# A fused attention, expert and gated kernel: the groups of small matmuls of two half-windows apart, and the loads placed otherwise in each slot

## The chip, the cores and the metric

The kernel runs on one core of a Trainium2 chip. The metric is the device time of one execution, in microseconds. Three runs of the kernel before took 1782.68, 1790.65 and 1793.02 us; the median is 1790.65 us. The profile is one more execution of its own.

## The reference

Three stages follow each other. Here they are, cut to what is computed:

```
q, k, v: (4, 8, 768, 48) float32, beta: (4, 8, 768)
# 1. delta-rule attention, for each of the 32 (batch, head) pairs, token after token
k_n = k / (norm(k) + 1e-6)
y[t]  = q[t] @ state
state = state + beta[t] * outer(k_n[t], v[t] - k_n[t] @ state)      # state is 48 x 48
# 2. x = y with heads side by side: (3072, 384); four experts, w1 (4,384,1024), w2 (4,1024,384)
p = domain_probs / (sum(domain_probs) + 1e-9)
x = sum over e of p[:, e] * (relu(x @ w1[e]) @ w2[e])
# 3. gated layer, w_gate and w_val (384,1536), w_out (1536,384)
out = (sigmoid(x @ w_gate) * (x @ w_val)) @ w_out
```

## The kernel before

**Windows and slots.** The attention stage doesn't go token by token. It takes chunks of 128 tokens (six of them) and half of the 32 heads at a time: 12 windows of 16 heads. Within a window the 128 steps of the recurrence become a triangular system for each head, and its inverse is built up from blocks of 32, then 64, then 128 rows. `slot(w, ...)` writes down one order of steps, and each engine (`@block.tensor`, `vector`, `scalar`, `gpsimd`) runs through the same list and takes from it the steps that it has work in. Engines meet only at semaphores, so the list fixes the order within each engine, and an engine that waits holds up everything behind it on that engine.

**What one slot holds.** Four kinds of work lie in slot w:

- `lev(step, w, p, hf)`: the triangular inverse of window w, for the half hf (8 heads). `first`, `y0` to `y3` and `z0` to `z3` are groups of matmuls on 32x32 blocks in float16 (lines 747 to 777), `m32y` and `m32z` (783 to 794) also, and `m64y`, `m64z` (802, 808) work on 64x64 blocks. A y group of one half is 32 matmuls; a z group is 4 wider ones and 32 small ones. After a y group VectorE masks the result (line 617), after a z group ScalarE copies it (line 531 is the common copy helper) and VectorE transposes it (line 602); the next group of that half needs both. `blocks` and `quads` are copies on GpSimd.
- `rec(step, w-1, ..., o)`: the recurrence of the window before, for the half o: `z`, `u0`, `au_a`, `au_b`, `u2`, `y`, `s` (float32 matmuls, lines 818 to 871).
- `pre(step, w+1, ...)`: the next window's norms, transposes (`turn`, line 879) and products (`product`, line 887); `product_q` is that of window w.
- `moe(step, m, ...)`, m = w-2: the first half of expert 0's hidden layer for the tokens that are done. `up` (line 934, nine matmuls 256 wide for one of four tiles f), ScalarE's Relu (line 595), VectorE's low part (`low`, line 711), `down` (line 943, three matmuls 384 wide for each f and each of two token tiles), and `weigh` (line 718), in which VectorE multiplies a finished tile by its expert weight into `part_out`. Where m is negative, four plain float16 matmuls stand in for each `up` and `down` (line 922).

`both(step)` runs a tile group for half 0 and then at once for half 1. So on TensorE the groups come in pairs: `y0` half 0, `y0` half 1, then the next piece of other work.

**Waits around the expert part.** `up(f)` uses one of two PSUM banks, f mod 2. For f below 2 it waits until `weigh(m-1, f)` has read that bank (`part_done`). In the list `weigh(m-1, 1)` stands after `both("z0")` and ahead of `au_a`, and `up(1)` after `au_a`. There is one `part_out` place: each `weigh` waits until the store of the one before has landed (`part_stored`).

**The DMA queue.** All transfers are issued by SyncE (SP) in one order, in a loop over w: `load_v`, the store of one weighed part, `load_k`, `load_b` (beta, spread over the partitions), at w = 2 the second half of expert 0's weights, the two stores of y, `load_x` (it waits for the y stores to land and reads them back for the expert part), `load_q`, and the store of the other weighed part. A `wait_ge` in that loop holds back all that follows it. `up(0)` waits for `load_x`.

**After the 12 slots** a tail finishes the last windows, and then the experts (lines 1050 to 1178) and the gated layer (lines 1308 to 1414) run. The change doesn't touch them.

Of the kernel before, what the change touches and what calls it, by code (L numbers as in the profile page):

```python
# [7 lines left out]
F32 = mybir.dt.float32  # L8
# [6 lines left out]
P = 128  # L15
# [52 lines left out]
def delta_rule_attention(nc, q, k, v, beta, consts, places, x_hi, x_lo, ident, id_in, early):  # L68
# [9 lines left out]
    with ctx:  # L78
        def sb(name, shape, dt=F32):
            return ctx.enter_context(nc.sbuf_tensor(name, shape, dt))  # L80
# [48 lines left out]
        w2h = [sb(f"w2half_{part}", [P, KH, KD * P], F32R) for part in "hl"]  # L129
        xs = [sb(f"xs_{part}", [P, KD, 2, P], F32R) for part in "hl"]  # L130
        hs = [sb(f"hs_{part}", [P, KH, 2 * P], F32R) for part in "hl"]
        part_out = sb("part_out", [P, KD * P])

        w_split = sem("w_split")
        p_in = sem("p_in")
# [67 lines left out]
        def slot(w, p, lev, rec, pre, moe):  # L203

            m, has_next = w - 2, w < NW - 1

            def r(step, o):
                if w > 0 and not (step == "s" and w == NW - 1):
                    rec(step, w - 1, 1 - p, o)

            def n(step, which=None):
                if has_next:
                    pre(step, w + 1, 1 - p, which)

            def both(step):
                for hf in range(2):
                    lev(step, w, p, hf)

            def down(window, t, *fs):
                for f in fs:  # L220
                    moe("down", window, t, f)

            def up(f):
                for part in range(2):
                    moe("up", m, f, part)

            pre("value", w, p, None)
            n("square")
            both("first")
            moe("weigh", m - 1, 0)  # L230
            r("u0", 0)
            down(m - 1, 1, 0, 1)
            r("u0", 1)
            both("y0")
            n("norm")
            down(m - 1, 1, 2, 3)
            up(0)
            n("unit", 0)
            n("unit", 1)
            both("z0")  # L240
            moe("weigh", m - 1, 1)
            r("au_a", 0)
            moe("low", m, 0)
            up(1)
            both("y1")
            r("au_b", 0)
            moe("low", m, 1)
            up(2)
            both("z1")
            r("au_a", 1)  # L250
            rec("z", w, p, 0)
            moe("low", m, 2)
            both("y2")
            n("turn", 0)
            r("au_b", 1)
            n("turn", 1)
            both("z2")
            r("u2", 0)
            rec("z", w, p, 1)
            both("y3")  # L260
            n("product", 0)
            r("u2", 1)
            both("z3")
            both("blocks")
            both("quads")
            r("y", 0)
            both("m32y")
            up(3)
            n("product", 1)
            both("m32z")  # L270
            moe("low", m, 3)
            r("y", 1)
            pre("product_q", w, p, 0)
            both("m64y")
            r("s", 0)
            down(m, 0, 0, 1)
            pre("product_q", w, p, 1)
            both("m64z")
            r("s", 1)
            down(m, 0, 2, 3)  # L280
            n("turn_q", 0)
            n("turn_q", 1)

        def run(lev, rec, pre, moe):
# [59 lines left out]
        with nc.Block() as block:  # L344

            @block.sync
            def _(sp):
# [4 lines left out]
                def load_k(w):  # L352
                    sp.dma_start(k_raw[w % 2][:, :, :], rows_of(k, w // 2, w % 2)).then_inc(k_in[w % 2], 16)

                def load_v(w):
                    sp.dma_start(v_raw[:, :, :], rows_of(v, w // 2, w % 2)).then_inc(v_in, 16)
# [35 lines left out]
                def store_part(m, o):  # L392
                    tok = first_token(m, o)
                    sp.wait_ge(part_done, 2 * m + o + 1)
                    sp.dma_start(early.part[tok:tok + P, :], part_out[:, :]).then_inc(part_stored[o], 16)

                load_k(0)
                sp.dma_start(ident[:, :], consts[2]).then_inc(id_in, 16)
# [7 lines left out]
                load_k(1)  # L406
                load_b(1)
                load_q(1)
                sp.dma_start(early.probs_raw[:, :, :], early.probs).then_inc(p_in, 16)
                early.load_first(sp)  # L410
                for w in range(NW):
                    if w + 1 < NW:
                        sp.wait_ge(vb_done, w + 1)
                        load_v(w + 1)
                    if 3 <= w:
                        store_part(w - 3, 1)
                    if w + 2 < NW:
                        sp.wait_ge(ku_done, 2 * (w + 1))
                        load_k(w + 2)
                        sp.wait_ge(kb_done, 2 * (w + 1))  # L420
                        load_b(w + 2)
                    if w == 2:
                        sp.wait_ge(w_split, 4)
                        early.load_second(sp)
                    if w:
                        store_y(w - 1, 0)
                        store_y(w - 1, 1)
                        load_x(w - 1)
                    if w + 2 < NW:
                        sp.wait_ge(tq_rdy, 2 * (w + 1))  # L430
                        load_q(w + 2)
                    if 2 <= w:
                        store_part(w - 2, 0)
                store_part(NW - 3, 1)
                store_part(NW - 2, 0)
                store_y(NW - 1, 0)
                store_y(NW - 1, 1)
                load_x(NW - 1)
                store_part(NW - 2, 1)
                for o in range(2):  # L440
                    store_part(NW - 1, o)
                for o in range(2):
                    sp.wait_ge(y_out[o], 64 * NW)
                    sp.wait_ge(part_stored[o], 16 * NW)
# [155 lines left out]
            def _(dve):  # L600
# [106 lines left out]
                def moe(step, m, f, part=1):  # L707
                    if step == "low" and m >= 0:
                        dve.wait_ge(hh_done, KH * m + f + 1)
                        past(dve, dn_rdy, 2 * m)  # L710
                        nc.vector.scalar_tensor_tensor(out=hs[1][:, f, :], in0=ebank[f % 2][:, 0:2 * P], scalar=0.0,
                                                       in1=hs[0][:, f, :].bitcast(F32), op0=ALU.max,
                                                       op1=ALU.subtract).then_inc(hl_done, 1)
                    if step == "weigh" and m >= 0:
                        tile = (2 * (m % 2) + f) * NCH + m // 2
                        dve.wait_ge(dn_rdy, 2 * m + f + 1)
                        past(dve, part_stored[1 - f], 16 * (m + f))
                        nc.vector.tensor_scalar(part_out[:, :], ebank[f][:, 0:KD * P],
                                                early.weights[:, tile, 0:1], None, ALU.mult).then_inc(part_done, 1)

                nc.vector.memset(XTf[:, :, :].bitcast(F32), 0.0).then_inc(x_zeroed, 1)
# [229 lines left out]
class Early:  # L951


    def __init__(self, nc, ctx, w1, w2, probs, halves_raw):
        E, D, F = w1.shape
        N = probs.shape[0]
        self.nc, self.kd, self.kh = nc, D // P, F // P // 2
        self.raw1 = halves_raw[:, 0:self.kd * F // 2].rearrange("p (t f) -> p t f", f=F // 2)
        self.raw2 = halves_raw[:, self.kd * F // 2:].rearrange("p (t d) -> p t d", d=D)
        self.w1, self.w2 = w1[0].rearrange("(t p) f -> p t f", p=P), w2[0].rearrange("(t p) d -> p t d", p=P)  # L960
        self.probs = probs.rearrange("(t p) e -> p t e", p=P)
        self.raw_in = ctx.enter_context(nc.semaphore("halves_in"))
        self.probs_raw = ctx.enter_context(nc.sbuf_tensor("pr", [P, N // P, E], F32))
        self.weights = ctx.enter_context(nc.sbuf_tensor("pn", [P, N // P, E], F32))
        self.sums = ctx.enter_context(nc.sbuf_tensor("psum_p", [P, N // P], F32))
        self.guarded = ctx.enter_context(nc.sbuf_tensor("prec", [P, N // P], F32))
        self.part = nc.dram_tensor("part", (N, D), F32, kind="Internal").ap()

    def load(self, sp, n):
# [7 lines left out]
    def load_second(self, sp):  # L977
        self.load(sp, 1)

    def normalize(self, dve, p_in, p_steps):  # L980
        nc, pr, pn = self.nc, self.probs_raw, self.weights
        dve.wait_ge(p_in, 16)
        nc.vector.reduce_sum(self.sums[:, :], pr[:, :, :], AX_X).then_inc(p_steps, 1)
        dve.wait_ge(p_steps, 1)
        nc.vector.tensor_scalar(self.guarded[:, :], self.sums[:, :], 1e-9, None, ALU.add).then_inc(p_steps, 1)
        dve.wait_ge(p_steps, 2)
        nc.vector.reciprocal(self.sums[:, :], self.guarded[:, :]).then_inc(p_steps, 1)
        dve.wait_ge(p_steps, 3)
        nc.vector.tensor_tensor(pn[:, :, :], pr[:, :, :], self.sums[:, :].unsqueeze(2).to_broadcast(pn.shape),
                                ALU.mult).then_inc(p_steps, 1)  # L990
        dve.wait_ge(p_steps, 4)

# [534 lines left out]
```

## Time and profile before

| | us |
|---|---|
| median of 3 runs | 1790.65 |
| lowest and highest | 1782.68, 1793.02 |
| the profiled execution, whole | 1771.93 |
| its span from first to last instruction | 1770.1 |
| TensorE (PE) busy | 1687.9 |
| PE weight load (PEld) busy | 1516.4 |
| VectorE (DVE) busy | 621.7 |
| ScalarE (ACT) busy | 443.8 |
| GpSimd (POOL) busy | 206.5 |

The profiled execution stands apart from the three timed ones and was faster than each. Busy time counts a matmul from its start to its modelled end, and matmuls overlap, so it is not a measure of progress. Starts are: the distance from the start of one group to the start of the next is the time that a group takes on PE. A lower granted clock makes the same work take longer, and the page shows it in tenths for 40 slices. "issue" as a releaser stands for time in which the engine waited for nothing that the profile shows.

### The profile page before, as it was taken

How to read it: one execution, taken by the hardware profiler on the slowest of the kernel's cores; microseconds unless marked ns; L12 is line 12 of the kernel's file. 1: busy time of each engine (PE TensorE's matmuls, PEld its weight loads, DVE VectorE, ACT ScalarE, POOL GpSimd, SP SyncE). 2: the span in 40 equal slices, each digit the busy share in tenths (PEclk: the TensorE clock that was granted, in tenths of full speed). 3: DMA queues.
4: the chain of work that ended last, by engine and by line, in shares of the span. 5: the costliest groups of instructions: out<-in, count | busy, mean ns of one | idle time of the engine just before them, and what ended most of it. 6: DMA issues, size and time to landing. Idle time of an engine off the chain costs nothing. (4 is left out here: it accounts for less than half of the span.)

```text
span 1770.1 us, 41908 instructions
## 1 busy us (share of the span) xinstructions
PE 1687.9 (95%) x18182; PEld 1516.4 (86%) x18182; DVE 621.7 (35%) x1169; ACT 443.8 (25%) x852; POOL 206.5 (12%) x309
## 2 busy tenths in 40 slices
PE   2899999999997799999999999999989999999999
PEld 2788899888987689999999999999978888888887
DVE  2565666565653223222222222222244222222222
ACT  2333333333331121221112111111133222222222
POOL 2522222222230030030002100000000000000000
PEclk9998999898998899999999999999999999999999
DMA  7143333333213734112122112112012000000000
GB/s 152 32 113 87 87 86 87 86 86 86 66 48 89 260 107 166 47 36 71 36 107 71 36 36 98 36 36 71 0 64 71 19 0 19 18 0 18 0 19 18
DMA packets 171757, 113.68 MB, mean 64 GB/s; under 512 B 82224, under 2 KB 151216, under 8 KB 171600
## 3 DMA queue, kind: packets, MB, share of 16 engines
q1 hardware_dynamic: 171600, 111.33, 22.1%
q8 instruction: 129, 2.11, 0.5%
q14 instruction: 28, 0.23, 0.0%
HBM read 92.44 MB, written 18.87 MB: 63 GB/s over the span
## 5 line engine op out<-in xcount | busy, mean ns | idle before, releaser
L1149 DVE SCALAR_TENSOR_TENSOR hl<-ebank,hh 128x512 fp32r<-128x512 f32 x168 | 116.3, 692 | 506.4 <-ACT hh L1114 506.4
L1114 ACT ACTIVATE hh<-ebank 128x512 fp32r<-128x512 f32 x168 | 100.6, 599 | 582.2 <-PE ebank L1178 582.2
L1176 PE MATMUL ebank<-w2l,hh 128*128 128x384 f32 x672 | 226.5, 337 | 2.6 <-DVE hl L1149 2.6
L1178 PE MATMUL ebank<-w2h,hh 128*128 128x384 f32 x672 | 226.6, 337 | 0.0
L1177 PE MATMUL ebank<-w2h,hl 128*128 128x384 f32 x672 | 225.9, 336 | 0.0
L1176 PE MATMUL ebank<-xl,w1h 128*128 128x512 f32 x504 | 197.2, 391 | 10.1 <-DMA xl<-x_lo 10.1
L1178 PE MATMUL ebank<-xh,w1h 128*128 128x512 f32 x504 | 199.7, 396 | 0.0
L1177 PE MATMUL ebank<-xh,w1l 128*128 128x512 f32 x504 | 199.5, 396 | 0.0
L1176 PEld LDWEIGHTS ebank<-w2l,hh 128*128 128x128 f32 x672 | 126.4, 188 | 9.8 <-DVE hl L1149 3.1
L1177 PEld LDWEIGHTS ebank<-w2h,hl 128*128 128x128 f32 x672 | 126.4, 188 | 6.0
L1178 PEld LDWEIGHTS ebank<-w2h,hh 128*128 128x128 f32 x672 | 126.3, 188 | 0.0
L1372 DVE TENSOR_TENSOR prod<-gbank,gate 128x512 f32<-128x512 f32 x72 | 49.7, 690 | 209.3 <-ACT gate L1319 209.3
L1176 PEld LDWEIGHTS ebank<-xl,w1h 128*128 128x128 f32 x504 | 95.4, 189 | 26.5 <-DMA xl<-x_lo 10.4
L1178 PEld LDWEIGHTS ebank<-xh,w1h 128*128 128x128 f32 x504 | 95.1, 189 | 20.4
L1177 PEld LDWEIGHTS ebank<-xh,w1l 128*128 128x128 f32 x504 | 95.2, 189 | 16.7
L1406 PE MATMUL gbank<-wol,mh 128*128 128x384 f32 x288 | 98.4, 342 | 0.7 <-DVE ml L1376 0.7
L1408 PE MATMUL gbank<-woh,mh 128*128 128x384 f32 x288 | 97.1, 337 | 0.0
L1407 PE MATMUL gbank<-woh,ml 128*128 128x384 f32 x288 | 96.8, 336 | 0.0
L1319 ACT ACTIVATE gate<-gbank 128x512 f32<-128x512 f32 x72 | 43.0, 598 | 208.6 <-PE gbank L1408 208.6
L1406 PE MATMUL gbank<-gxl,wgh 128*128 128x512 f32 x216 | 84.8, 393 | 4.4 <-DVE gxl L1366 4.4
L1408 PE MATMUL gbank<-gxh,wgh 128*128 128x512 f32 x216 | 86.2, 399 | 0.0
L1407 PE MATMUL gbank<-gxh,wgl 128*128 128x512 f32 x216 | 86.0, 398 | 0.0
(160 smaller groups left out, 2914.9 us busy)
## 6 DMA issues: line engine op xcount, KB each, us to landing
xh<-x_hi SPq DMA_DIRECT2D x24, 768.0 KB, 4.4
xl<-x_lo SPq DMA_DIRECT2D x24, 768.0 KB, 6.0
brep<-in_beta SPq DMA_DIRECT2D x24, 256.0 KB, 5.4
k_raw<-in_k SPq DMA_DIRECT2D x12, 384.0 KB, 4.5
v_raw<-in_v SPq DMA_DIRECT2D x12, 384.0 KB, 4.5
q<-in_q SPq DMA_DIRECT2D x12, 384.0 KB, 5.7
x_hi<-yhi SPq DMA_DIRECT2D x48, 96.0 KB, 2.1
x_lo<-ylo SPq DMA_DIRECT2D x48, 96.0 KB, 2.2
```

The source lines that it names most:

```text
L1114: nc.scalar.activation(hs[i][0][:, :], bank[i][:, :], ACT.Relu).then_inc(hh_done, 1)
L1149: nc.vector.scalar_tensor_tensor(out=hs[i][1][:, :], in0=bank[i][:, :], scalar=0.0, in1=hs[i][0][:, :].bitcast(F32), op0=ALU.max, op1=ALU. ...
L1176: mm(dst, stat[0], mov[1], start=first, stop=False)
L1177: mm(dst, stat[1], mov[0], start=False, stop=False)
L1178: return mm(dst, stat[0], mov[0], start=False, stop=last)
L1319: nc.scalar.activation(gate[:, :], bank[f % 2][:, :], ACT.Sigmoid).then_inc(gate_done, 1)
L1372: nc.vector.tensor_tensor(prod[:, :], bank[2 + f % 2][:, :], gate[:, :], ALU.mult)\
L1406: mm(dst, stat[0], mov[1], start=first, stop=False)
L1407: mm(dst, stat[1], mov[0], start=False, stop=False)
L1408: return mm(dst, stat[0], mov[0], start=False, stop=last)
```

## The change

The pairs of tile groups are taken apart: behind each half stands a piece of other work. `weigh`, `low`, `norm` and `product` keep their places between the same groups as far as that goes, and so `weigh(m-1, 1)` now stands behind `z0` of half 1 and directly ahead of `up(1)`. `part_out` has two places, one for each half, and the scratch of the weight normalization lies in it. SP's loop has a new order. The diff, without the lines that only rename the normalization's scratch:

```
-        part_out = sb("part_out", [P, KD * P])
+        part_out = sb("part_out", [P, 2, KD * P])
+        early.room(part_out[:, :, :].rearrange("p t d -> p (t d)"))
...
-            def both(step):
-                for hf in range(2):
-                    lev(step, w, p, hf)
+            def tiles(step, hf):
+                lev(step, w, p, hf)
...
             n("square")
-            both("first")
+            tiles("first", 0)
+            r("u0", 0)
+            tiles("first", 1)
             moe("weigh", m - 1, 0)
-            r("u0", 0)
             down(m - 1, 1, 0, 1)
             r("u0", 1)
-            both("y0")
+            tiles("y0", 0)
+            down(m - 1, 1, 2, 3)
+            tiles("y0", 1)
             n("norm")
-            down(m - 1, 1, 2, 3)
             up(0)
             n("unit", 0)
             n("unit", 1)
-            both("z0")
+            tiles("z0", 0)
+            r("au_a", 0)
+            tiles("z0", 1)
             moe("weigh", m - 1, 1)
-            r("au_a", 0)
             moe("low", m, 0)
             up(1)
-            both("y1")
+            tiles("y1", 0)
             r("au_b", 0)
+            tiles("y1", 1)
             moe("low", m, 1)
             up(2)
-            both("z1")
+            tiles("z1", 0)
             r("au_a", 1)
+            tiles("z1", 1)
             rec("z", w, p, 0)
             moe("low", m, 2)
-            both("y2")
+            tiles("y2", 0)
             n("turn", 0)
             r("au_b", 1)
+            tiles("y2", 1)
             n("turn", 1)
-            both("z2")
+            tiles("z2", 0)
             r("u2", 0)
+            tiles("z2", 1)
             rec("z", w, p, 1)
-            both("y3")
+            tiles("y3", 0)
             n("product", 0)
+            tiles("y3", 1)
             r("u2", 1)
-            both("z3")
-            both("blocks")
-            both("quads")
+            tiles("z3", 0)
             r("y", 0)
-            both("m32y")
+            tiles("z3", 1)
+            tiles("blocks", 0)
+            tiles("blocks", 1)
+            tiles("quads", 0)
+            tiles("quads", 1)
             up(3)
+            tiles("m32y", 0)
             n("product", 1)
-            both("m32z")
+            tiles("m32y", 1)
             moe("low", m, 3)
             r("y", 1)
+            tiles("m32z", 0)
             pre("product_q", w, p, 0)
-            both("m64y")
+            tiles("m32z", 1)
             r("s", 0)
             down(m, 0, 0, 1)
+            tiles("m64y", 0)
             pre("product_q", w, p, 1)
-            both("m64z")
+            tiles("m64y", 1)
             r("s", 1)
-            down(m, 0, 2, 3)
+            down(m, 0, 2)
+            tiles("m64z", 0)
+            down(m, 0, 3)
             n("turn_q", 0)
+            tiles("m64z", 1)
             n("turn_q", 1)
...
                 for w in range(NW):
-                    if w + 1 < NW:
-                        sp.wait_ge(vb_done, w + 1)
-                        load_v(w + 1)
+                    if w:
+                        store_y(w - 1, 0)
                     if 3 <= w:
+                        store_part(w - 3, 0)
                         store_part(w - 3, 1)
                     if w + 2 < NW:
                         sp.wait_ge(ku_done, 2 * (w + 1))
                         load_k(w + 2)
+                    if w + 1 < NW:
+                        sp.wait_ge(vb_done, w + 1)
+                        load_v(w + 1)
+                    if w:
+                        store_y(w - 1, 1)
+                    if w + 2 < NW:
                         sp.wait_ge(kb_done, 2 * (w + 1))
                         load_b(w + 2)
-                    if w == 2:
-                        sp.wait_ge(w_split, 4)
-                        early.load_second(sp)
                     if w:
-                        store_y(w - 1, 0)
-                        store_y(w - 1, 1)
                         load_x(w - 1)
                     if w + 2 < NW:
                         sp.wait_ge(tq_rdy, 2 * (w + 1))
                         load_q(w + 2)
-                    if 2 <= w:
-                        store_part(w - 2, 0)
-                store_part(NW - 3, 1)
-                store_part(NW - 2, 0)
+                    if w == 2:
+                        sp.wait_ge(w_split, 4)
+                        early.load_second(sp)
+                for o in range(2):
+                    store_part(NW - 3, o)
                 store_y(NW - 1, 0)
                 store_y(NW - 1, 1)
                 load_x(NW - 1)
-                store_part(NW - 2, 1)
-                for o in range(2):
-                    store_part(NW - 1, o)
+                for m in (NW - 2, NW - 1):
+                    for o in range(2):
+                        store_part(m, o)
...
                     if step == "weigh" and m >= 0:
...
-                        past(dve, part_stored[1 - f], 16 * (m + f))
-                        nc.vector.tensor_scalar(part_out[:, :], ebank[f][:, 0:KD * P],
+                        past(dve, part_stored[f], 16 * m)
+                        nc.vector.tensor_scalar(part_out[:, f, :], ebank[f][:, 0:KD * P],
```

## Rows read from the trace of the kernel before

**Rows 1.** The page: engine totals, and the queue that carries instructions (packets, MB).

```profile
PE 1687.9 (95%) x18182; PEld 1516.4 (86%) x18182; DVE 621.7 (35%) x1169; ACT 443.8 (25%) x852; POOL 206.5 (12%) x309
...
q8 instruction: 129, 2.11, 0.5%
```

**Rows 2.** Windows, one for each of slots 2 to 10: stretch, busy, PEclk, DMA, GB/s.

```profile
core 0: us, PE busy (x) PEld busy (x) DVE busy (x) ACT busy (x) POOL busy (x), PEclk, DMA share, GB/s
114.52:160.45 45.93, 43.72 (x1034) 39.71 (x1033) 26.11 (x58) 16.42 (x36) 11.43 (x21) 0.89 0.44 112
...
284.74:325.38 40.64, 39.94 (x1029) 36.62 (x1028) 26.45 (x60) 16.14 (x36) 11.45 (x21) 1.00 0.41 92
325.38:372.15 46.77, 44.53 (x1030) 40.66 (x1029) 26.66 (x60) 16.25 (x36) 11.45 (x21) 0.89 0.38 86
...
413.23:460.57 47.34, 45.63 (x1030) 41.61 (x1030) 26.86 (x60) 16.47 (x36) 11.45 (x21) 0.86 0.34 80
460.57:501.21 40.64, 39.97 (x1030) 36.66 (x1030) 26.45 (x60) 16.14 (x36) 11.45 (x21) 1.00 0.29 67
sum 386.69, PE 374.35 PEld 341.92 DVE 238.49 ACT 145.94 POOL 103.04; mean PE 41.59 PEld 37.99 DVE 26.50 ACT 16.22 POOL 11.45
```

**Rows 3.** Waits of PE and its weight loads, 50 to 560 us: total, times, longest.

```profile
PE bank L934 <- DVE part_out L718: 4.4, 9, 0.5
...
PEld bank L887 <- DVE QK L704: 4.3, 11, 0.6
```

**Rows 4.** Timeline of PE in slot 4, groups merged: start, length, engine, line.

```profile
209.60 0.29 PE L772 MATMUL bank<-XX,c 32*32 32x256 f16 x4
...
210.02 0.29 PE L772 MATMUL bank<-XX,c 32*32 32x256 f16 x4
...
210.46 1.09 PE L841 MATMUL bank<-U,A 128*128 128x48 f32 x8
212.04 0.39 PE L934 MATMUL bank<-xs_l,w1half_h 128*128 128x256 f32 x1 [0.49 <-DVE part_out L718]
...
213.30 0.67 PE L763 MATMUL bank<-XX,Ah 32*32 32x32 f16 x64
213.89 1.09 PE L844 MATMUL bank<-U,A 128*128 128x48 f32 x8
...
222.79 1.07 PE L852 MATMUL bank<-R,XTf 128*128 128x48 f32 x8
223.70 1.11 PE L818 MATMUL bank<-S,KQ 128*128 128x96 f32 x8
...
226.43 1.07 PE L852 MATMUL bank<-R,XTf 128*128 128x48 f32 x8
227.44 0.29 PE L772 MATMUL bank<-XX,c 32*32 32x256 f16 x4
```

**Rows 5.** Timeline of PE in slot 0: a y half standing alone.

```profile
43.34 0.40 PE L763 MATMUL bank<-XX,Ah 32*32 32x32 f16 x32 [0.36 <-DVE XX L610]
43.67 3.59 PE L922 MATMUL bank<-c 128*128 128x256 f16 x16
```

**Rows 6.** Timeline of VectorE in slot 4, ahead of `up(1)`.

```profile
210.70 0.79 DVE L602 STREAM_TRANSPOSE XX<-XX 128x256 f16<-128x256 f16 x2 [1.80 <-ACT XX L531]
211.41 0.58 DVE L718 TENSOR_SCALAR part_out<-bank,pn 128x384 f32<-128x384 f32 x1
```

**Rows 7.** Timeline of PE: the longest stalls of slots 2, 7 and 9.

```profile
134.35 0.26 PE L772 MATMUL bank<-XX,c 32*32 32x256 f16 x1 [2.03 <-issue]
...
341.31 0.18 PE L777 MATMUL bank<-Yc,XX 32*32 32x32 f16 x1 [1.57 <-issue]
...
431.69 0.98 PE L844 MATMUL bank<-U,A 128*128 128x48 f32 x7 [1.04 <-issue]
```

**Rows 8.** Windows, columns as in Rows 2, ahead of the stall in slot 7.

```profile
336.00:340.00 4.00, 3.74 (x154) 3.38 (x152) 1.79 (x5) 1.15 (x3) 0.00 (x0) 1.00 0.91 202
```

**Rows 9.** Timeline of SP: a load issue of slot 7, and the x loads around slot 5's start.

```profile
335.64 1.98 SPq L366 DMA_DIRECT2D brep<-in_beta  x2
...
243.38 0.91 SPq L389 DMA_DIRECT2D xs_h<-x_hi  x2
```

More of the change, by code:

```diff
@@ L394, in store_part @@
                     sp.wait_ge(part_done, 2 * m + o + 1)
-                    sp.dma_start(early.part[tok:tok + P, :], part_out[:, :]).then_inc(part_stored[o], 16)
+                    sp.dma_start(early.part[tok:tok + P, :], part_out[:, o, :]).then_inc(part_stored[o], 16)
                 load_k(0)
@@ L408, in _ @@
                 load_q(1)
-                sp.dma_start(early.probs_raw[:, :, :], early.probs).then_inc(p_in, 16)
+                sp.dma_start(early.probs_raw, early.probs).then_inc(p_in, 16)
                 early.load_first(sp)
                 for w in range(NW):
-                    if w + 1 < NW:
-                        sp.wait_ge(vb_done, w + 1)
-                        load_v(w + 1)
+                    if w:
+                        store_y(w - 1, 0)
                     if 3 <= w:
+                        store_part(w - 3, 0)
                         store_part(w - 3, 1)
@@ L962, in __init__ @@
         self.raw_in = ctx.enter_context(nc.semaphore("halves_in"))
-        self.probs_raw = ctx.enter_context(nc.sbuf_tensor("pr", [P, N // P, E], F32))
         self.weights = ctx.enter_context(nc.sbuf_tensor("pn", [P, N // P, E], F32))
-        self.sums = ctx.enter_context(nc.sbuf_tensor("psum_p", [P, N // P], F32))
-        self.guarded = ctx.enter_context(nc.sbuf_tensor("prec", [P, N // P], F32))
         self.part = nc.dram_tensor("part", (N, D), F32, kind="Internal").ap()
@@ L978, in load_second, with room @@
         self.load(sp, 1)
+    def room(self, scratch):
+        n, e = self.weights.shape[1:]
+        self.probs_raw = scratch[:, 0:n * e].rearrange("p (n e) -> p n e", e=e)
+        self.sums, self.guarded = scratch[:, n * e:n * e + n], scratch[:, n * e + n:n * e + 2 * n]
     def normalize(self, dve, p_in, p_steps):
@@ L982, in normalize @@
         dve.wait_ge(p_in, 16)
-        nc.vector.reduce_sum(self.sums[:, :], pr[:, :, :], AX_X).then_inc(p_steps, 1)
+        nc.vector.reduce_sum(self.sums, pr, AX_X).then_inc(p_steps, 1)
         dve.wait_ge(p_steps, 1)
-        nc.vector.tensor_scalar(self.guarded[:, :], self.sums[:, :], 1e-9, None, ALU.add).then_inc(p_steps, 1)
+        nc.vector.tensor_scalar(self.guarded, self.sums, 1e-9, None, ALU.add).then_inc(p_steps, 1)
         dve.wait_ge(p_steps, 2)
-        nc.vector.reciprocal(self.sums[:, :], self.guarded[:, :]).then_inc(p_steps, 1)
+        nc.vector.reciprocal(self.sums, self.guarded).then_inc(p_steps, 1)
         dve.wait_ge(p_steps, 3)
-        nc.vector.tensor_tensor(pn[:, :, :], pr[:, :, :], self.sums[:, :].unsqueeze(2).to_broadcast(pn.shape),
+        nc.vector.tensor_tensor(pn[:, :, :], pr, self.sums.unsqueeze(2).to_broadcast(pn.shape),
                                 ALU.mult).then_inc(p_steps, 1)
```

## The prediction

> **What bounds the kernel now.** I first read the page's totals and then cut the attention stage into its slots. PE is busy for 95% of the span [rows 1], but ends of matmuls are modelled, so I read starts. By slots [rows 2], the reader is to see that the bare slot lasts 40.64 us (slots 6 and 10, PEclk 1.00), that its 1029 matmuls follow each other nearly without a hole, and that DVE (26.5), ACT (16.1) and POOL (11.5) have slack. So a slot is the sum of what PE does, and whatever the change adds to PE is paid in full. The nine slots together take 386.69 us, and nine bare ones would take 365.76: 20.9 us are disturbance, and 18.1 of them lie in three slots, 45.93, 46.77 and 47.34 us long, with a mean clock of 0.89, 0.89 and 0.86. The timeline shows in each of those a stall put down to "issue", of 2.03, 1.57 and 1.04 us [rows 7], and the slots' low clock comes after it. The stall is of the kind that late instructions would give: the page has 129 transfers of instructions, 2.11 MB or 16 KB each [rows 1], and ahead of the stall in slot 7 the DMA engines were 0.91 busy [rows 8] with the load of k and beta issued some 3.7 us before [rows 9]. Last, the table of waits [rows 3] names two small regular ones, on `weigh` (9 times, 0.5 us at most) and on QK's mask (11 times, 0.6 at most).
>
> **The change, part by part.**
>
> *Thirteen pairs of tile groups taken apart.* The same matmuls run, but the array goes between small tiles and full width 13 more times per slot, in and out. Both edges have a price in the starts. A pair of y groups takes 213.89 - 213.30 = 0.59 us [rows 4]; one alone took 0.33 [rows 5], two are 0.66: +0.07. In a z pair the first half takes 0.42 (210.02 - 209.60) and the second, which goes over to wide work, 0.44 [rows 4]: +0.02. And the piece put between ends before tiles: the same eight `u2` matmuls take 0.91 us ahead of wide work and 1.01 ahead of tiles [rows 4]: +0.10. So a split y costs 0.17 and a split z or `first` 0.12. Four y, four z, `first`: 0.68 + 0.48 + 0.12 = 1.28 us. For `m32y`, `m32z`, `m64y`, `m64z` I have no single half; between 0.02 (z's own edge) and 0.17, and since they are bare groups as y is, 0.13 each, 0.5 together. Some pieces put between (`product`, `y` of the recurrence) are followed by another shape in both orders, so that about four of the 0.10 fall away: -0.4. I take 1.4 us per slot. Bounds: 0.4 if only y's and z's trailing edges counted (4 x 0.07 + 5 x 0.02), 13 x 0.17 = 2.2 if each cost the most. Twelve slots: 17 us (5 to 26).
>
> The Trainium skill (TensorEngine Tiling (Array Packing), Tiling Modes, Key Properties) says that changing the tiling mode drains the TensorE, while going from tile to tile in one mode does not. The trace agrees, with 0.10 us at the one edge; the rule speaks against this change, and the sum by it has the same sign and no other size.
>
> *`weigh(m-1, 1)` and `up(1)`.* Now `z0`'s second half ends at 210.46, its copy and transposes run, `weigh` starts at 211.41 and takes 0.58, and `up(1)` starts at 212.04 [rows 4, 6]: 1.58 us after `z0`, on ScalarE's copy, VectorE's transpose and `weigh` in turn. `au_a` lies in that time and covers 0.93 (as many matmuls, `u2`, take 0.91), so PE loses 0.65. In the new order `au_a` stands between the halves, `weigh` still stands behind the transpose of half 1 on VectorE, and `up(1)` comes straight behind `z0` half 1. The chain of 1.58 stays and has no cover: PE loses 1.58 less the usual 0.10 to a next group, 1.48. That is +0.83 us in the nine slots that weigh something, +7.5. What waits behind it: `up(1)` holds all of PE's queue. Bounds: 0 if the two places made `weigh` earlier, which I exclude, since the wait is for the transposes ahead of it and not for a store; +1.0 if the copy also slips.
>
> *Two places for the parts.* They take away `weigh`'s wait for the store of the other half. In steady slots the row puts the wait on the mask, not the store, so: nothing, 0 to 0.5 us in the tail, where the last `weigh` waits for the store ahead. I take -0.5 once. *QK's mask:* `m64y` half 0 now stands ahead of the second `product_q`, which hides that wait: 4.3 us over 11 slots [rows 3], of which half is a load of weights that is anyway not on the path: -2 (0 to -4).
>
> *SP's order.* k, v, beta leave the first half of the slot (in slot 7 the last of these started 10.3 us behind the slot's start [rows 9, 2]) and follow the stores of y. All are needed a slot later or more, except v, which GpSimd multiplies at the end of the slot and which is not read until 16 us on. The one that could bite is `load_x`, which `up(0)` waits for. It was issued at 243.38, 0.6 us ahead of slot 5 [rows 9]. It now stands behind the beta load, whose two issues take 1.98 us [rows 9]; but SP sat waiting for the y stores to land in that place, and with four more pieces of PE work behind the recurrence's `y`, its own start moves ahead of the slot's end by some 2 us. I take 0, bounds -0.5 and +1.5 per slot. `load_second` moves behind them, for the experts far later: 0.
>
> *What the quiet first half gives.* If the stalls in slots 2, 7 and 9, with the low clock behind them, come from loads that hold up instructions, they go: 18.1 us, and most of the 2.8 in the other slots: -20 in this execution. Bounds: 0, and -21 for the profiled execution. Breaking up the pairs also spreads the densest runs of instructions, which helps the same stalls.
> The Trainium skill (Runtime: NRT & Kernel Launch, Instruction fetch mechanics) says that instructions come in 16 KiB blocks, and that the cost of crossing into a next one is mostly hidden. By that rule moving the loads gives 0. The size agrees with the page's 129 transfers; stalls of 1.0 to 2.0 us speak against "hidden" here.
>
> *Sum.* 17 + 7.5 - 0.5 - 2 = +22 added for certain, -20 from the stalls: +2 against the profiled execution's 1771.93, or 1774. The timed runs lie 18.7 above that execution. I can't see why; more stalls and low clock of the same kind are the nearest reason, and then they shrink as well. I let a quarter of the 18.7 go, -5: 1790.65 + 2 - 5 = 1788 us.
>
> **The rivals.**
>
> *Everything of that kind goes.* All 20.9 and all of the 18.7 are load-made: 1790.65 + 22 - 39 = 1774 us. For it: the long stalls lie 16 to 18 us into a slot, behind k's and beta's loads. Against it: slots 6 and 10 had the same loads and no stall.
>
> *The stalls stay (slower).* PE simply eats its instructions faster than they come in `z1` to `y3`, whatever the loads do. One mechanism, in that stretch, priced by the stalls' remaining: 1790.65 + 22 = 1813 us, and it decides from the point at which less than 4 of the 22 are won back elsewhere. For it: the stall in slot 9 is there with beta's load mostly over; the total count of instructions is unchanged.
>
> *The clock (much slower).* Behind the stalls the clock fell in stretches without a hole of their own. The change thins just that stretch with edges, and 1.5 us of nothing at `up(1)`. A disturbed slot lost about 6 us, some 4.4 of it clock (6.1 less the stall's 1.6 in slot 7). If the clock fell in half of the slots that now hold: 5 x 4.4 more and none won back, 1790.65 + 22 + 22 = 1835 us.
>
> *The change doesn't do what it says.* `load_x` and `load_q` stand last, and run over into the next slot as now; if the edges cost only the lower bound (5 us) and `up(1)`'s chain shortens, 1790.65 + 5 - 2 - 25 = 1769 us.
>
> **How the numbers follow.** My forecast, most stalls go and the edges cost what the starts say, gets 0.40, with a range of its own from 1779 to 1799. All gone 0.22; stalls stay 0.22; clock 0.08; cheap edges 0.08. The range from 1770 to 1816 leaves out the clock and a part of the cheap edges and of "all gone". Less than 0.5% (9 us) is no change that a measurement of this kernel tells: 1781.7 to 1799.6. Faster: 0.06 of mine, 0.19 of all gone, 0.07 of cheap edges: 0.32. Same: 0.28 of mine and 0.04: 0.32. Slower: 0.06 of mine, 0.22, 0.08: 0.36.
>
> **What would show it.** In the windows of bare slots of the kernel after, 42.5 to 43.5 us instead of 40.64 with PEclk 1.00. In the timeline a hole of about 1.5 us ahead of `up(1)` in each slot from 3 on, with `weigh` as its releaser; single y groups of 0.33 and z groups of 0.44 us. In the waits, no L887 on QK, and "issue" with no entry over 1 us. In the windows, a DMA share near zero from 6 us to 28 us into a slot. I am wrong if bare slots stay under 41.5 us, if the longest "issue" stalls are still there with the engines idle, or if `up(0)` waits for x.

## The result, and the profile after

The changed kernel takes 1845.03 us (median of 4 runs, 1831.32 to 1851.95) against 1786.66 us (4 runs of the kernel before, 1775.64 to 1793.02). The ratio is 1.031, with a 95% interval from 1.026 to 1.037: slower by 3.1%. I had forecast 1788 us and a range up to 1816.

The page of the kernel after: engine totals, and the granted clock of TensorE in 40 slices.

```profile
PE 1766.1 (95%) x18182; PEld 1575.8 (85%) x18182; DVE 625.0 (34%) x1169; ACT 443.6 (24%) x852; POOL 205.7 (11%) x309
...
PEclk9997787797678879999999999999999999999999
```

The same 18182 matmuls are busy for 78 us longer [rows 1], at the same 95%. From 700 us on the clock is full, as before. The profiled execution took 1851.95 us, the longest of the four runs, and is 80.0 us above that of before, where the medians differ by 58.4; what follows are the microseconds of these two traces. By starts, the experts begin at 675.59 us instead of 593.19 (+82.4), and all behind them takes 2 us less. So the whole loss lies in the attention stage. Cut into slots (windows, one for each of slots 2 to 10; some of them and the sum; columns as in [rows 2]):

```profile
111.47:152.60 41.13, 41.01 (x1033) 36.39 (x1032) 25.64 (x58) 16.01 (x36) 11.37 (x21) 1.00 0.40 86
152.60:208.26 55.66, 54.03 (x1029) 48.04 (x1028) 26.96 (x60) 16.44 (x36) 11.40 (x21) 0.72 0.40 96
...
315.53:367.11 51.58, 49.95 (x1030) 44.56 (x1030) 26.87 (x60) 16.23 (x36) 11.41 (x21) 0.80 0.33 70
367.11:413.92 46.81, 44.48 (x1029) 39.48 (x1029) 26.66 (x60) 16.01 (x36) 11.40 (x21) 0.93 0.37 81
...
466.27:522.27 56.00, 54.23 (x1029) 48.09 (x1028) 26.96 (x60) 16.44 (x36) 11.40 (x21) 0.73 0.33 73
...
sum 463.58, PE 447.22 PEld 397.72 DVE 240.55 ACT 146.02 POOL 102.59; mean PE 49.69 PEld 44.19 DVE 26.73 ACT 16.22 POOL 11.40
```

The reader is to see the step between the first two lines. Slot 2, the last in which no part is weighed, is 41.13 us long at full clock, with all pairs apart and the new loads. Slot 3 is the first with a `weigh`, and it and all after it are 46.8 to 56.0 us long, at 0.72 to 0.93. The nine slots take 463.58 us where 386.69 stood [rows 2]: 76.9 of the 82.4.

What changes from slot 2 to 3 is one wait. The timeline of the kernel after in slot 6: PE from `z0` of half 0, then VectorE, then what PE does behind it.

```profile
322.88 0.39 PE L796 MATMUL bank<-Yc,XX 32*32 32x32 f16 x32
323.20 1.09 PE L860 MATMUL bank<-U,A 128*128 128x48 f32 x8
324.22 0.29 PE L791 MATMUL bank<-XX,c 32*32 32x256 f16 x4
324.34 0.39 PE L796 MATMUL bank<-Yc,XX 32*32 32x32 f16 x32
326.25 0.39 PE L953 MATMUL bank<-xs_l,w1half_h 128*128 128x256 f32 x1 [1.51 <-DVE part_out L737]
...
327.81 1.84 PE L863 MATMUL bank<-U,A 128*128 128x48 f32 x8
```

```profile
325.25 0.45 DVE L621 STREAM_TRANSPOSE XX<-XX 128x256 f16<-128x256 f16 x1 [0.95 <-ACT XX L550]
325.62 0.58 DVE L737 TENSOR_SCALAR part_out<-bank,pn 128x384 f32<-128x384 f32 x1
```

`up(1)` starts 2.03 us after `z0` of half 1 began, of which 0.45 is the group itself (in e8 below, where `up(1)` doesn't wait, it starts 0.45 behind): the chain of 1.58 us that the prediction read from [rows 4, 6], now bare. The eight matmuls at 327.81 then take 1.77 us until the next group, tiles, where such a group took 1.01 ahead of tiles [rows 4]. Windows of the same slot show it:

```profile
315.53:324.50 8.97, 8.85 (x247) 8.11 (x250) 5.39 (x15) 3.29 (x8) 3.00 (x4) 1.00 0.79 147
324.50:328.00 3.50, 1.99 (x79) 1.73 (x59) 1.29 (x4) 0.77 (x2) 0.63 (x1) 0.99 0.00 0
328.00:348.40 20.40, 20.40 (x353) 18.64 (x352) 8.25 (x18) 4.16 (x9) 0.00 (x0) 0.50 0.01 3
348.40:367.11 18.71, 18.71 (x386) 16.08 (x385) 11.94 (x24) 8.02 (x17) 7.77 (x17) 1.00 0.52 119
```

Full clock, a hole, and then 20.4 us at 0.50, in which PE counts as busy without a break. That is the lower of the two clock levels (1.2 GHz). It comes in all nine slots from 3 to 11 and in none of slots 1 and 2.

### The profile page after: what moved, and what is told of

The parts are those of the page before. It is cut to its first block and busy times, and to the rows that moved or that the text cites. A ratio compares the mean times of both kernels' runs of the same rounds, so it can differ in the third digit from the quotient of the medians.

```text
span 1850.2 us, 41907 instructions
## 1 busy us (share of the span) xinstructions
PE 1766.1 (95%) x18182; PEld 1575.8 (85%) x18182; DVE 625.0 (34%) x1169; ACT 443.6 (24%) x852; POOL 205.7 (11%) x309
## 5 line engine op out<-in xcount | busy, mean ns | idle before, releaser
L1199 PEld LDWEIGHTS ebank<-xh,w1l 128*128 128x128 f32 x504 | 94.9, 188 | 16.7
```

Source lines behind the costliest of these rows:

```text
L1199: mm(dst, stat[1], mov[0], start=False, stop=False)
```

## The experiments

All are timed against the kernel before, run beside them, and the ratio is to that. Its median was 1786.6 us beside e1 to e4, 1796.6 beside e5, e6, e8 and e9, 1791.7 beside e10 and e11, and 1793.3 beside e12, so across these groups the ratios compare and the microseconds only roughly. The interval behind a ratio is its 95% interval.

**e1: the wait taken away, all else of the change kept.**

```
-            tiles("z0", 1)
             moe("weigh", m - 1, 1)
+            tiles("z0", 1)
```

> The changed kernel with one line moved: VectorE's second weigh (m-1, 1) stands ahead of z0 of half 1 in the list, not behind it, so that up(1) no longer waits for z0's copy, transpose and weigh in turn. All 13 pairs stay apart, the loads stay where the change puts them. Theory H (the 1.6 us hole ahead of up(1) brings the low clock of slots 3 to 11): hole and low clock both go, slots fall from some 53 us to about 41.2, time 1750 to 1770 us. Rival E (the edges of the 13 split pairs thin the stretch y1 to z3, and that alone brings the low clock): only the hole goes, 9 x 1.5 = 13 us, so about 1832 us, granted clock of slots 3 to 10 still near 0.8.

Measured: 1761.4 us, ratio 0.983 (0.974 to 0.992). Windows of its slots 4 and 6:

```profile
194.12:238.10 43.98, 41.66 (x1029) 37.03 (x1028) 26.63 (x60) 16.00 (x36) 11.41 (x21) 1.00 0.43 97
...
279.99:321.86 41.87, 41.63 (x1031) 37.04 (x1030) 26.65 (x60) 16.02 (x36) 11.40 (x21) 1.00 0.42 91
```

One line moved gives 84 us back (1845.0 - 1761.4, each from its own comparison), and nine waits of 1.5 us are 14 of them. The clock is 1.00 in all of slots 2 to 10. The split pairs by themselves don't lower it: E falls, H stands.

**e4: the wait put into the kernel before, pairs and loads untouched.**

```
+            r("au_a", 0)
             both("z0")
             moe("weigh", m - 1, 1)
-            r("au_a", 0)
```

> The kernel before with one step moved: au_a of half 0 stands ahead of the z0 pair and not behind weigh, so that nothing covers the chain z0, copy, transpose, weigh ahead of up(1). Pairs and loads are as before. Theory H: a hole of 1.5 us where 0.65 was, and the clock low behind it in slots 3 to 11, 1787 + 8 + 9 x 8 to 11 = 1865 to 1890 us. Rival E (edges are what matters): the hole alone, 9 x 0.85 = 8 us, 1795 us, clock as before.

Measured: 1812.21 us, ratio 1.015 (1.011 to 1.020). Its waits, and its slots 4 and 5:

```profile
PE bank L934 <- DVE part_out L718: 13.6, 9, 1.5
```

```profile
214.44:267.84 53.40, 51.06 (x1029) 46.49 (x1029) 26.87 (x60) 16.46 (x36) 11.46 (x21) 0.74 0.32 72
267.84:312.19 44.35, 42.44 (x1031) 38.90 (x1030) 26.65 (x60) 16.14 (x36) 11.45 (x21) 0.92 0.38 87
```

Where the wait was 4.4 us in all [rows 3] it is 13.6, and some 26 us are lost where the length explains 9. (The execution with this profile took 1836.47 us, 24 above the median, so its trace shows more low clock than the median goes with.) In slots 3 and 8 the clock held behind the hole and fell 11 and 15 us later, behind issue stalls of 1.66 and 0.68 us; in the other six it fell behind the hole. So the hole lowers the clock in pairs too, but not every time, and my 1865 to 1890 was far too high. By the trace's records of the granted clock it stayed low for 10.2 us or less in five of the eight slots 3 to 10; in the changed kernel it stays low for 20 us and more in seven of these eight.

**e9: the wait kept, PE given idle work in it.**

```
+                        if f == 1 and part == 0 and 1 <= m <= NW - 3:
+                            pe.wait_ge(u0_done, 2 * m + 4)
+                            for _ in range(12):
+                                mm(rbank[1][:, 0:2 * P], eye, small_eye, start=True, stop=True)
                         if part == 0 and f < 2:
```

> The changed kernel, complete, with twelve idle float16 matmuls (128 x 256, into a bank whose content is no longer needed) ahead of up(1) in the slots that weigh a part: PE waits as long as before, but works meanwhile. Nothing that is computed changes. Theory H (what the hole costs is the low clock behind it, and an idle PE is what brings that): the clock of slots 3 to 11 stays full and the time comes to e1's plus the hole, 1761 + 9 x 1.5 = 1775 us. Rival (the wait itself, or what lies around it, delays the work behind it, and the clock only follows): no gain, about 1845 us.

Measured: 1778.98 us, ratio 0.989 (0.985 to 0.994). PE in slot 3, and the windows of slots 3 and 6:

```profile
164.13 0.39 PE L796 MATMUL bank<-Yc,XX 32*32 32x32 f16 x32
164.46 1.49 PE L949 MATMUL bank<-c 128*128 128x256 f16 x12
166.04 0.39 PE L957 MATMUL bank<-xs_l,w1half_h 128*128 128x256 f32 x1
```

```profile
154.40:198.58 44.18, 43.19 (x1041) 38.21 (x1040) 26.67 (x60) 16.00 (x36) 11.39 (x21) 1.00 0.46 112
286.41:330.62 44.21, 43.10 (x1041) 38.18 (x1040) 26.66 (x60) 16.01 (x36) 11.41 (x21) 1.00 0.39 86
```

`up(1)` starts 1.91 us after `z0`'s small matmuls began (166.04 - 164.13), the same 1.91 as in the changed kernel (326.25 - 324.34). The wait is all there; only its idleness is gone, and with it 66 us by the medians (1845.0 - 1779.0) and some 75 by the ratios (1.031 against 0.989). This is the experiment that shows the cause: PE idle at this place, not late work.

These slots are 44.2 us long where e1's 41.9 and the wait of 1.4 make 43.3; the rest is an issue stall early in the slot (0.77 us in slot 3, 0.90 in slot 6). Seven of the eight slots from 3 to 10 have one, of 0.7 to 1.4 us, and behind one of them alone, the 1.30 us in slot 9, the clock fell, for 6.8 us.

**e11: half of it filled** (six instead of twelve).

> e9 with six idle matmuls instead of twelve, so that about half of the hole ahead of up(1) is idle (0.85 us) in each slot from 3 on. Theory H with a size: the kernel before has a hole of 0.65 us at this place without the clock falling behind it, e4 and the changed kernel one of 1.58 us with it. If 0.85 us is harmless as 0.65 was: clock full, 1775 to 1780 us, as e9. If it is enough: the clock falls in some slots, 1800 to 1845 us. A theory in which only the length of the chain counts, idle or not, expects e9's time here too.

Measured: 1789.60 us, ratio 0.997 (0.993 to 1.001). Slot 9, and then slot 10, the only one of slots 3 to 10 with a low clock:

```profile
414.59:457.85 43.26, 42.39 (x1035) 37.55 (x1034) 26.67 (x60) 16.01 (x36) 11.40 (x21) 1.00 0.38 84
457.85:515.73 57.88, 56.18 (x1037) 49.39 (x1036) 26.97 (x60) 16.45 (x36) 11.40 (x21) 0.71 0.28 62
```

An idle rest of 0.75 us is harmless in the seven slots from 3 to 9. In slot 10 an issue stall came first, 6 us into the slot. PE and a window behind the stall:

```profile
465.36 0.36 PE L957 MATMUL bank<-xs_l,w1half_h 128*128 128x256 f32 x1 [1.48 <-issue]
...
469.15 1.46 PE L949 MATMUL bank<-c 128*128 128x256 f16 x6
```

```profile
467.30:468.60 1.30, 1.30 (x12) 1.21 (x15) 0.45 (x1) 0.29 (x1) 0.14 (x1) 0.56 0.00 0
```

The clock was already low when the idle matmuls began at 469.15, so the half-filled wait has no part in this fall; the low clock then lasted 34.1 us. The median lies between the two times that I expected, 0.8% above e9 by the ratios or 14 us, which is about what this one slot costs (57.88 - 43.26 = 14.6).

**e2: the old order of the loads, the rest as changed.**

> The changed kernel with SP's loop in its old order (the two places for the weighed parts kept). Theory H: hole and low clock unchanged, 1845 us give or take 10, with a few issue stalls back. Rival L (the new order of the loads is itself the cause of the low clock, through late data): about 1800 us, the low clock of slots 3 to 11 gone.

Measured: 1864.86 us at the median, but its four runs lie from 1824.88 to 1865.43, too far apart for a ratio; three of them are within 1 us of each other. The median is 10 us above the range that I gave. In its trace slots 6 and 7 are 51.55 and 54.27 us at 0.80 and 0.75, and the records of the granted clock have it low for 20 us and more in each slot from 3 to 11. Rival L falls: the new order of the loads isn't what lowers the clock there.

**e3: the new order of the loads and two places alone,** the list of before.

> The kernel before with the new order of SP's loop and two places for the weighed parts, the slot's list as before. If the long issue stalls of the kernel before come from loads in the first half of the slot: they and the low clock behind them go, 1765 to 1772 us, slots 2 to 10 at 40.6 to 41 us. If they come from the density of instructions alone: no change, 1787 us, with stalls over 1 us in the trace. Rival L: slower than before, over 1800 us.

Measured: 1780.43 us, ratio 0.988 (0.978 to 0.997). Better than before, but not by my reason: slots 2 to 10 are 42.1 to 47.4 us long. PE and the window of slot 4:

```profile
205.80 0.34 PE L947 MATMUL bank<-w2half_h,hs_h 128*128 128x384 f32 x1
208.12 0.36 PE L938 MATMUL bank<-xs_l,w1half_h 128*128 128x256 f32 x1 [1.98 <-issue]
```

```profile
200.27:246.38 46.11, 43.95 (x1029) 40.14 (x1029) 26.57 (x60) 16.13 (x36) 11.41 (x21) 0.89 0.36 84
```

The issue stalls that stood 14 to 18 us into a slot [rows 7] now stand 4 to 7 us into it, in all nine slots from 2 to 10 (0.64 to 2.16 us, six of them over 1 us), where x and q are now on their way (in slot 4 issued from 200.70 to 202.7).

**e5: e1 with the pairs together again** (weigh ahead of the pair, new loads).

> e1 with the pairs put back together: the list of the kernel before with weigh (m-1, 1) ahead of the z0 pair, the new order of the loads and two places. Against e1 it shows what the 13 split pairs do by themselves. If they only cost their edges (1.2 us a slot as e1's bare slots of 41.9 say against 40.6 less 0.65): e5 is faster than e1, 1750 us. If spreading the instructions out spares the issue stalls that e3 has 4 to 7 us into a slot: e5 keeps those stalls and their low clock, about 1772 us, slower than e1.

Measured: 1787.25 us, ratio 0.996 (0.993 to 1.000), where e1 had 0.983: by the ratios 1.3% slower, some 24 us, in spite of fewer edges. Its PE in slot 6, with the window around it:

```profile
289.20 0.34 PE L947 MATMUL bank<-w2half_h,hs_h 128*128 128x384 f32 x1
291.90 0.55 PE L938 MATMUL bank<-xs_l,w1half_h 128*128 128x256 f32 x1 [2.36 <-issue]
```

```profile
288.00:292.00 4.00, 1.64 (x39) 1.31 (x29) 2.99 (x10) 0.33 (x2) 2.33 (x3) 0.92 1.20 220
```

In slots 2 to 10 of e5 seven issue stalls are over 1 us, the longest 2.54, and in e1 one is, of 2.04. Splitting the pairs is what makes these stalls rare; it was the useful half of the change. (e5 differs from e3 only in `weigh`'s place, and their intervals overlap.)

**e6: e1 with the old loads.**

> e1 with the old order of the loads (two places kept). If the new order is worth what e3 showed (0.5 to 1%): 1772 us. If the split pairs alone spare the stalls, wherever the loads lie: 1761 us, as e1. If the stalls at 14 to 17 us into a slot come back with their low clock: 1780 us.

Measured: 1774.31 us, ratio 0.989 (0.985 to 0.993). Five of its slots (4 and 7 to 10) are near bare, 41.9 to 42.2 us, and one has a stall of 1.53 us 16.7 us into it and is then 50.4 us long at 0.83. The old order alone thus leaves stalls where they were, fewer with the pairs apart; by the times e6 and e1 can't be told apart, as their intervals overlap.

**e8: `weigh` one step further up, ahead of both `z0` halves.**

> e1 with weigh (m-1, 1) one step further up, ahead of z0 of half 0. In e1 up(1) still starts 0.63 us after z0 half 1, where 0.45 is usual, so 9 x 0.18 = 1.6 us are to be had: 1760 us, which the comparison will hardly tell from e1. If VectorE is late with z0's transposes instead, a wait appears ahead of z0 and it is slower than e1 by a few us.

Measured: 1760.71 us, ratio 0.982 (0.978 to 0.986); not to be told from e1. Its bare slot is 41.70 us, e1's 41.87.

**e10: e8 with k, v and q issued from `u2` on, x last.**

```
+                    if w:
+                        sp.wait_ge(u_done, 2 * w)
...
+                    if w + 2 < NW:
+                        sp.wait_ge(tq_rdy, 2 * (w + 1))
+                        load_q(w + 2)
                     if w:
                         store_y(w - 1, 0)
...
                     if w:
                         load_x(w - 1)
-                    if w + 2 < NW:
-                        sp.wait_ge(tq_rdy, 2 * (w + 1))
-                        load_q(w + 2)
```

> e8 with SP's loop in a third order: from u2 of the recurrence on (some 28 us into the slot) load_k, load_v and load_q, then y's first store, the parts, y's second store, beta, and x last. So the traffic that is left over into the next slot is x alone. If the issue stalls of 0.6 to 1.0 us that e8 and e1 still have some 6 us into a slot come from x's, beta's and q's traffic there: they go, slots at 41.7 us, 1756 us, at the edge of what the comparison tells. If they come from the density of the instructions there: no change, 1761 us. If q's traffic at 30 us delays y's stores and so x: up(0) waits for x, 1765 us or more.

(The new places of `load_k` and `load_v` lie in the lines left out.) Measured: 1756.60 us, ratio 0.979 (0.974 to 0.983), the lowest of all, though its interval overlaps those of e8 and e1. Windows of slot 3 and, in three pieces, slot 6:

```profile
153.33:195.01 41.68, 41.56 (x1030) 37.04 (x1029) 26.68 (x60) 16.01 (x36) 11.41 (x21) 1.00 0.49 125
```

```profile
278.46:286.46 8.00, 7.88 (x213) 7.20 (x213) 5.07 (x15) 3.07 (x8) 2.04 (x3) 1.00 0.49 112
286.46:305.00 18.54, 18.54 (x531) 16.97 (x532) 12.19 (x27) 6.25 (x14) 1.59 (x2) 1.00 0.02 4
305.00:320.14 15.14, 15.14 (x295) 12.86 (x289) 9.41 (x19) 6.69 (x15) 7.77 (x17) 1.00 0.88 191
```

The eight slots from 3 to 10 are 41.68 to 41.76 us long, and in these eight no issue stall is over 0.5 us. This is what "loads in the second half" can give; the change's own order had left x and q over.

**e12: e10 with pairs.**

> e10 with the pairs of tile groups put back together (weigh (m-1, 1) ahead of the z0 pair, loads in e10's order, two places). The edges of the 13 split pairs cost 1.7 us a slot (bare slots of 41.7 us in e10, of 40.0 in e5 when the issue stall is taken off). If the issue stalls of pairs come only where load traffic lies (14 to 17 us into the slot in the kernel before, 4 to 7 in e3 and e5), they are gone with e10's order, and this is the fastest of all: 1756 - 12 x 1.7 = 1736 us. If pairs make stalls by their density alone, they remain, with low clock behind them: 1760 to 1780 us, and splitting the pairs is what pays.

Measured: 1765.18 us, ratio 0.984 (0.979 to 0.990). Slot 3 and slot 10, and PE's longest stall:

```profile
154.69:206.77 52.08, 49.73 (x1030) 45.63 (x1030) 26.89 (x60) 16.24 (x36) 11.42 (x21) 0.77 0.41 104
456.76:496.74 39.98, 39.80 (x1029) 36.61 (x1029) 26.61 (x60) 16.14 (x36) 11.42 (x21) 1.00 0.27 65
```

```profile
164.73 0.19 PE L783 MATMUL bank<-Yc,XX 32*32 32x32 f16 x4 [2.18 <-issue]
```

A bare slot of pairs is 39.98 us, the shortest seen, so the edges of 13 split pairs cost 41.68 - 39.98 = 1.7 us. In the traces stalls and low clock eat more than that: slots 3 to 10 take 342 us here and 334 in e10. By the timed runs the two kernels can't be told apart, as the intervals overlap. The transfers ahead of this stall are mainly the expert weights of `load_second`, issued once, from 154.86 on, 0.2 us into the slot. e10 issued them 1.7 us ahead of its slot 3 and had no stall. The first windows of slot 3, of e12 and then of e10:

```profile
154.69:160.69 6.00, 5.88 (x167) 5.59 (x167) 4.33 (x10) 2.57 (x6) 2.03 (x2) 1.00 1.07 318
```

```profile
153.33:159.00 5.67, 5.55 (x137) 5.08 (x136) 3.41 (x7) 2.52 (x6) 1.92 (x2) 1.00 1.10 337
```

Traffic of the same density, a stall from 7.9 to 10.0 us into the slot with pairs, and none with the pairs apart. It is one stall in one trace. Slot 5 of e12 shows another thing: no wait of PE in it is over 0.3 us, and still the clock fell, 20 us into the slot:

```profile
267.40:277.70 10.30, 10.30 (x186) 9.46 (x186) 4.65 (x10) 2.35 (x4) 1.88 (x5) 0.50 0.22 46
```

## Why the prediction was wrong

I forecast about no change (1788 us against 1790.65), and measured 3.1% more. The parts that only cost were seen; what one of them does to the clock was not. Point by point:

- **The step that failed is "`weigh(m-1, 1)` and `up(1)`".** It found the wait, its nine slots and its size: 1.58 us of chain. But it priced an idle PE by the length of the idleness, +7.5 us, and bounded that at +1.0 a slot. The kernel before already had 0.65 us at this place (0.49 as the waits count it, where they have 1.51 now) with full clock behind it, and I took the 1.58 to be of the same kind. e9 shows what it costs beyond its length: 66 us by the medians, some 75 by the ratios, with the same wait. In the trace after, slots 3 to 10 take 422.5 us against 346 for eight slots of e1's 41.9 plus 1.4 us of wait; some 3 us are issue stalls, the other 73 the clock.
- **The clock rival** named this place and stretch, and gave 1835, within the runs measured. It had 0.08. It was priced with the low spells of before (4.4 us lost in each; 6.1 less 1.6 is 4.5) in five slots; there were nine, and in slots 3 to 10 each lost some 9 us (73 / 8), twice that. The trace of before held the warning: three slots with a stall over 1 us and no other cause had a low clock behind them [rows 7, 2]. I used these to price a gain and not to price a hole that I had myself computed for every slot.
- **The edges:** 1.4 us a slot forecast, 1.7 measured (a bare slot of e10 against one of e12). Right mechanism, a little small, and not all in the places that I gave: a y half alone takes 0.30 us (e1, starts at 290.57 and 290.87), half of the pair's 0.59, and so has no edge of its own, where I took 0.33 from [rows 5]. The Trainium skill (TensorEngine Tiling (Array Packing), Tiling Modes) has the drain at a change of mode; the trace agrees with the existence of a cost, 0.13 us for each of the 13.
- **QK's mask:** the -2 was a misreading. The 4.3 us of [rows 3] are waits of the weight loads; PE itself waited 0.3 us for this mask in the kernel before and 0.2 in the kernel after.
- **SP's order:** x was on time but for one wait of 0.3 us. (A small misreading: beta's load was issued 4.1 us ahead of slot 7's stall, 341.31 - 1.57 - 335.64, and not 3.7.) That the loads' traffic would make stalls where it now lies, early in the slot, I had not seen: e3 lost there most of what it won. The -20 was half right. With pairs apart and the traffic truly out of the way, e10 wins all of it: its eight slots hold no disturbance.
- **Two places for the parts:** forecast at -0.5; what they are worth isn't shown, as no experiment took them alone.
- **"The stalls stay"** fell as a cause (density alone): with pairs apart and x and q out of the way (e10), slots 3 to 10 showed no stall over 0.5 us, and under the dense traffic of `load_second` it was the kernel with pairs that stalled (e12). So density seems to have its part, together with traffic. The Trainium skill (Runtime: NRT & Kernel Launch, Instruction fetch mechanics) calls the crossing to the next 16 KiB block mostly hidden. The traces agree for e10's slots and not for the others, with stalls up to 2.5 us. That they go with the transfers of instructions can be read from the traces: slots 1 to 11 of the thirteen traces hold 15 issue stalls over 1.5 us, and ahead of each a 16 KB transfer on the instruction queue starts 0.4 to 1.9 us before it (in e12 at 162.16, the stall at 162.55). Only 28% of all moments from 110 to 500 us have one so near. Whether PE waits for just these instructions, and whether the loads delay them, isn't shown.

What stays open: why the same hole costs 20 us and more of low clock in seven of eight slots with split pairs, and 10.2 us or less in five of eight with pairs (e4). Open too is why e1's slot 4 carried an issue stall of 2.0 us 6 us into the slot with no low clock behind it, when 1.5 us idle at 9 to 11 us did harm in every slot of the changed kernel. What follows differs (`up(0)` and `up(1)`, wide work, in the first case; `y1` to `z3`, small groups, in the second), but no experiment moved the hole alone. And in slot 5 of e12 the clock fell without a hole. So idle time is shown as the cause at this place; how much of it lowers the clock, and where, is not.

## What to carry to other kernels

When a step is moved so that PE waits bare for a chain over ScalarE and VectorE, price the idle PE by what the clock did behind the holes already in the trace, not by the hole's length: here 1.5 us idle in each of nine slots cost 7 to 8 us a slot more than itself (66 to 75 us in all). Read the busy share and the granted clock together, since at half clock PE shows as fully busy. A load moved out of a dense stretch has to be followed to where its traffic then lies.

## What was not expected of the hardware

- Behind an idle 1.58 us the granted clock fell to 0.50 and stayed there for 20.4 us in slot 6 (6.8 to 30.7 us in slots 3 to 10, by the records of the granted clock), with PE busy all along.
- Twelve float16 matmuls on constants, 1.49 us of work thrown away, kept the clock up in seven of the eight slots from 3 to 10 (the eighth has 6.8 us of low clock), and took the kernel from 1845 to 1779 us (ratios 1.031 and 0.989).
- With the new order of the loads, the kernels with pairs had six (e3) and seven (e5) issue stalls over 1 us in slots 2 to 10, up to 2.54 us; with a piece of wide work between the halves there was one in e1 (2.04 us) and one in the changed kernel (1.30 us), and in e10's slots 3 to 10 none over 0.5 us.
- All 15 issue stalls over 1.5 us have a 16 KB transfer of instructions that starts 0.4 to 1.9 us ahead of them.
